# Opening of a banded attention + two-layer product kernel: the halves of v 0 later, the maxima of v shifted by a unit, w_in's transfer one pair earlier in the queue

## The reference, cut to what matters

```python
# attention: batch 2, heads 8, sequence 768, head width 64; n_global 8, n_local 96
scores = scale * q @ k.T + bias            # bias: -slope(head) * distance
scores = where(is_global | is_local, scores, -1e9)   # local: 0 <= row-col < 96; global: col < 8
a = softmax(scores);  x = a @ v            # fp32
x = reshape(x, (1536, 512))
h = x @ w_in (512 x 2048); g = h * tanh(softplus(h)); x = g @ w_out (2048 x 512)
p = domain_probs / sum(domain_probs)
out = sum over 4 experts e of p[:, e] * (relu(x @ w1[e]) @ w2[e])   # w1: 512 x 1024
```

## Time and profile before

| | us |
|---|---|
| median of 3 runs | 901.03 |
| lowest, highest | 900.47, 902.30 |
| the profiled execution's own time | 900.44 |
| its span in the trace | 898.5 |
| busy: PE, DVE, ACT, POOL | 872.5, 482.7, 319.0, 260.9 |

### The profile page before, as it was taken

The page is one execution under the profiler, slowest core; times in us unless marked ns, Lnnn a source line. Parts: engine busy times, 40 slices in busy tenths (PEclk is TensorE's granted clock), DMA queues, the critical chain, the costliest instruction groups (busy, mean ns, idle before and its releaser), DMA issues.

```text
span 898.5 us, 12643 instructions
## 1 busy us (share of the span) xinstructions
PE 872.5 (97%) x4918; PEld 444.0 (49%) x4918; DVE 482.7 (54%) x1008; ACT 319.0 (35%) x596; POOL 260.9 (29%) x222
## 2 busy tenths in 40 slices
PE   6988999999999999999999999999999999999998
PEld 5766876444444444444444444444444444444443
DVE  7756887999999989874442125222134321212121
ACT  4898886545554655542021010102010111101020
POOL 1659992222222222210039200077000292000000
PEclk8988999999999999999999999999999999999999
DMA  9961510000000000202100500001300000000001
GB/s 213 307 209 37 168 59 1 1 1 1 1 7 4 0 1 1 97 1 94 10 1 0 187 1 1 6 0 63 124 1 7 0 0 0 0 24 23 35 12 49
DMA packets 52004, 39.19 MB, mean 44 GB/s; under 512 B 40816, under 2 KB 41712, under 8 KB 51440
## 3 DMA queue, kind: packets, MB, share of 16 engines
q1 hardware_dynamic: 49888, 34.31, 12.9%
q10 hardware_dynamic: 2064, 4.19, 1.3%
HBM read 35.35 MB, written 3.15 MB: 43 GB/s over the span
## 4 chain that ended last, share of the span: by engine, by line
PE 89%; ACT 5%; DVE 3%; issue 1%; SPq 1%; DMA 0%; POOL 0%; DVEq 0%
PE bank L615 68%; PE bank L687 14%; PE bank L548 2%; PE bank L586 2%; ACT scaled L872 2%; PE bank L605 2%; ACT tmp L858 1%; ACT tmp L897 1%; PE bank L503 1%; DVE xT L1219 1%; SPq L420 1%; DMA xT<-in_v 0%; DVE tmp L1122 0%; ACT hid L848 0%; DVE tmp L1234 0%
## 5 line engine op out<-in xcount | busy, mean ns | idle before, releaser
L966 ACT ACTIVATE hid<-bank 128x512 f16<-128x512 f32 x96 | 57.3, 597 | 422.2 <-PE bank L615 422.2
L615 PE MATMUL bank<-xT,wA 128*128 128x512 f16 (+1 forms) x864 | 194.7, 379 | 0.0
L1344 DVE SCALAR_TENSOR_TENSOR hid<-bank,hid 128x512 f16<-128x512 f32 x96 | 66.4, 692 | 181.7 <-ACT hid L966 181.7
L615 PEld LDWEIGHTS bank<-xT,wA 128*128 128x128 f16 x864 | 84.4, 98 | 100.6
L687 PE MATMUL bank<-hid,wB 128*128 128x512 f16 x576 | 132.2, 379 | 0.9 <-DVE xT L1219 0.9
L615 PE MATMUL bank<-xT,wB 128*128 x576 | 125.3, 379 | 0.0
L615 PE MATMUL bank<-wB,hid 128*128 128x512 f16 x576 | 125.3, 379 | 0.0
L615 PE MATMUL bank<-wA,hid 128*128 128x512 f16 x576 | 125.3, 379 | 0.0
L824 POOL TENSOR_TENSOR tmp<-tmp 128x512 f32<-128x512 f32 x48 | 61.5, 1281 | 189.9 <-DVE tmp L1367 189.9
L781 POOL TENSOR_SCALAR stage<-stage,sc 128x1024 f32<-128x1024 f32 x32 | 36.0, 1125 | 260.4 <-DVEq L1337 250.4
L1424 DVE SCALAR_TENSOR_TENSOR acc<-bank,pg,acc 128x512 f32<-128x512 f32 x36 | 27.0, 750 | 131.7 <-PE bank L615 131.7
(11 more groups left out here) (113 smaller groups left out, 949.1 us busy)
## 6 DMA issues: line engine op xcount, KB each, us to landing
stage<-in_moe_w SPq DMA_DIRECT2D x8, 2048.0 KB, 9.8
stage<-in_moe_w_in SPq DMA_DIRECT2D x1, 4096.0 KB, 14.5
wB<-in_moe_w_out ACTq DMA_DIRECT2D x1, 4096.0 KB, 16.4
hid<-in_q SPq DMA_DIRECT2D x16, 192.0 KB, 3.4
hid<-in_k SPq DMA_DIRECT2D x16, 192.0 KB, 3.6
xT<-in_v SPq DMA_DIRECT2D x8, 384.0 KB, 5.1
out_y<-acc SPq DMA_DIRECT2D x12, 256.0 KB, 2.0
rows<-max SPq DMA_DIRECT2D x4, 128.0 KB, 4.3
```

Source lines behind the costliest of these rows:

```text
L615: last = pe.matmul(dst, lhs(c, a), rhs(c, b), start=(c == 0 and n == 0), stop=(c == chunks - 1 and n == 2))
L966: act.activation(hv[:, f, 0, :], psum(f % 4), ACT.Relu).then_inc(f_hi, 1)
L1344: dve.scalar_tensor_tensor(hv[:, f, 1, :], psum(f % 4), 0.0, hv[:, f, 0, :], ALU.max, ALU.subtract).then_inc(f_ready, 1)
```

## The change

Four things change; the arithmetic stays the same.

1. ACT's `values_high()` moves from ahead of pair 0 into unit 0 of pair 0, behind the high half of unit 0's P and the exponential of unit 2.
2. DVE's `values_low()` moves from ahead of pair 0 into unit 1, behind the low half of unit 1's P.
3. The maxima of v 1, 2, 4, 6 move from (ahead of pair 0, unit 1, unit 3, unit 5) to units 2, 3, 4 and 5.
4. SP issues w_in and the probabilities behind q and k of pair 2, ahead of those of pair 3.

```diff
         V_SUMS = list(range(3, PAIRS, 2))
+        V_MAX_AT = {2: 1, 3: 2, 4: 4, 5: 6}
+        VALUES_LOW_AT = 1
...
             for n in range(2, PAIRS):
                 sp.wait_ge(tr_psum, FILLS * (n - 1))
                 load_pair(n // 2, n % 2)
-                if n == 3:
+                if n == 2:
                     sp.dma_start(stage[:].rearrange("p (c f) -> p c f", c=DC), w_in_d).then_inc(w_loaded, 16)
...
                 if banded:
                     expo(0, 0, 0, banded)
                     expo(0, 0, 1, banded)
-                values_high()
+                else:
+                    values_high()
...
                     at = (2 * i + slot) * UNITS + u
+                    if banded and at == 0:
+                        values_high()
...
-            def value_step(u):
-
-                n = u + 1
-                if n < PAIRS and n not in V_SUMS:
+            def value_step(u, banded):
+
+                if banded and u == VALUES_LOW_AT:
+                    values_low()
+                if u in V_MAX_AT:
+                    n = V_MAX_AT[u]
                     dve.wait_ge(v_loaded[n], 16)
...
                 elif u + 1 == PAIRS:
-                    dve.wait_ge(v_pairs_max, PAIRS - 1 - len(V_SUMS))
+                    dve.wait_ge(v_pairs_max, len(V_MAX_AT))
...
-                value_step(0)
-                values_low()
-                pair(0, 0, is_banded, lambda u: u and value_step(u))
+                if not is_banded:
+                    values_low()
+                pair(0, 0, is_banded, lambda u: value_step(u, is_banded))
```

## The result

The changed kernel takes 906.94 us (median of 8 runs, 901.87 to 909.75), the kernel before 900.58 beside it (8 runs). The ratio is 1.0060, 95% interval 1.0046 to 1.0074: slower, by 6.4 us between the medians and 5.5 between the means. The forecast was 899.5, and the range (898.4 to 903.8) does not hold the time. The profiled execution took 906.68 with a span of 904.7, 6.2 longer than that of before.

What follows compares the result with a forecast made beforehand. PE, busy 97% of the span, was taken to bound the kernel, with engines in order so that opening savings reach the end. Opening -1.5 and w_in 0 on 901.03 gave 899.5 us, range 898.4 to 903.8.

Steps and rivals of the forecast that it cites:

- What bounds the kernel, and that opening time reaches the end: Whole kernel: PE busy 97%, engines in order; microseconds saved in the opening reach the end unless a transfer or POOL is late.
- The opening, -1.5: Pairs 0 and 1: reordering v 0's halves and the maxima saves 1.5 us, a little below the computed 1.73.
- timetable: Computed schedule of PE, ACT and DVE, unit 0 of pair 0 to pair 1's end: last unit 1.73 us early.
- w_in, 0: SP's queue: moving w_in and the probabilities ahead of pair 3's q and k was costed at 0 us.
- w_in through at 36.3, the probabilities at 37.5: SP's queue: times in us by which these transfers, issued from 24.3, would be through, before pair 3's packets.
- queued well ahead of w_out: SP's queue: pair 3's q and k are issued before w_out, so their possible 1.5 us loss was taken as 0.
- SP can keep the queue full: SP's queue: pair 2's transfers were taken to show this, as an argument against late q and k; no size.
- Some 1350 packets left at 39.2: Pair 3's packets when w_out's begin; sharing with w_out, they land near 47.7, past the allowed 46.2: 1.5 us lost.
- pair 3's q and k come late: Main rival, at pair 3's first fill: transfers stuck behind w_out land around 51; +3.3 us, 904.3; chance 0.25.
- most of its signs in the trace: Idle of several us before the fill near 45, ended by q or k; SP standing on L420 with w_out under way.
- The Trainium skill's rule: DMA engines alternate between queues by the packet, so small packets behind a second queue starve; it speaks against the change.

Runs made afterwards that it cites:

- e1: Parts 1 to 3 of the change on the kernel before, w_in and the probabilities back behind pair 3's q and k: 899.44 us for 901.19, ratio 0.9980.
- e8: The opening alone (parts 1 to 3 on the kernel before) repeated on another chip: 900.41 us for 900.89, ratio 0.9992.
- e11: The kernel before, unchanged, traced once more on another chip to see how it starts; no run time given.
- e12: The kernel before, unchanged, traced yet again to see how it starts; no run time given.
- e5: Parts 1 and 2 alone on the kernel before: v 0's halves moved, the maxima where they were; 902.25 us for 900.78, ratio 1.0008.
- e6: Part 3 alone on the kernel before: the maxima moved, v 0's halves still ahead of pair 0; 901.24 us for 900.78, ratio 1.0004.
- e2: Part 4 alone on the kernel before: w_in and the probabilities ahead of pair 3's q and k; 901.62 us for 901.19, ratio 1.0006.
- e3: The changed kernel with w_out issued four units later on ACT: 899.89 us where the kernel before has 901.19, ratio 0.9983.
- e4: The changed kernel with the probabilities back behind pair 3's q and k, only w_in ahead: 901.06 us where the kernel before has 901.19, ratio 1.0002.
- e10: The opening alone with 14 instead of 26 filler matmuls on PE ahead of the first fill: 900.99 us where the kernel before has 900.89, ratio 0.9995.

## Why the prediction was wrong

**What bounds the kernel, and that opening time reaches the end: right.** In e1's trace 1.5 us at pair 2's first fill (31.32 for 32.85) were still 1.5 at the first matmul group of w_out (165.69 for 167.20). A slow stretch of clock near 60 us can hide this: e8 is as early as e1 at pair 3's first fill (45.41), but has one and reaches w_out only at 167.37. The two traces of before that have one too (e11, e12) are there at 168.66, 1.3 later.

**The opening, -1.5: about right as a sum, wrong in its split.** Over the six traces that have the whole opening and all the fillers the scale of v comes at 28.25 to 28.96, over four that have the old one at 29.59 to 29.78, about 1.3 us apart; the runs give 1.25. The length of the wait at the first `pv` (1.92 us, timetable 1.9) and the order of the steps were as forecast. Wrong was that each part alone would give something: the timetable let e5 and e6 gain 0.6 and 0.4, they gained nothing.

**w_in, 0: wrong, and this is the step that failed.** The sum behind it had three terms, and I took its borderline result as nothing.
- w_in through at 36.3, the probabilities at 37.5: near enough. Most packets of the probabilities moved between 36 and 38.
- Pair 3's transfers "queued well ahead of w_out", since "SP can keep the queue full": this failed. I took it that q and k stand in the queue behind w_in and flow at 1040 packets per us once it is through. In fact SP was held 10.74 us on the second q and issued both k's at 38.28 and 38.87, level with w_out. The trace of before had a warning: SP's 9.07 us on two k's with w_out under way. It is not quite the same case, for there w_in was through and the 4 MB stood in ACT's queue. What the two have in common is that nothing or little of SP's small transfers moved while SP stood. I used that row for the rival and did not ask what it means for issues behind w_in.
- Some 1350 packets left at 39.2: it was both k's and most of the second q, about 2100. And they did not share from 39.2: SP's queue moved none from 41 to 43. So the last one landed at 54.7, not 47.7, and the loss was 9.4 us (54.76 for 45.36 in e1), not 1.5.

**The rival "pair 3's q and k come late" was right in its direction, its place (the fill near 45) and most of its signs in the trace.** Its way there was another: it let SP be stuck on the k's behind w_out, and landing at 51. SP was stuck on the second q behind w_in, before w_out was issued, and the k's themselves were issued in 0.55 and 0.84 us. I gave it 0.25 and priced it at +3.3; it was +6.4. The runs of the changed kernel spread from 901.87 to 909.75, those of the opening alone (e1 and e8) from 899.12 to 901.42 in 22. e2 with 0.8 us of start had 1.0 us of wait, e3 with 6.9 none. That the spread of single runs comes from how the race between 38.28 (k) and 38.31 (w_out) falls is argued from these, not traced.

**The Trainium skill's rule** ("DMA: Bandwidth & Descriptors", section "Queues, rings and completion order": the DMA engines take turns between queues by the packet) is what the trace after shows, 170 packets against 169. Two things beside it made the loss: SP stood while a large transfer was ahead in its queue, and for some 3 us SP's packets did not move at all behind a w_out just issued. The trace of before has that too: at 43:44, with SP's k's waiting, only w_out's queue moved.

```profile
q10 hardware_dynamic: 190, 0.39, 102.8%
```

**Left open.** What holds SP. e4 shows it is not the probabilities alone, since without them it stands 9.20 us one transfer later. A plain limit on the packets that wait in the queue does not fit both: e4 was held at the issue that makes 2304 packets behind w_in, the changed kernel passed 2304 (1536 of the probabilities, 768 of the first q) after 2.17 us and was held at 3072. In both, the one held is the third transfer issued behind w_in; no run here tests whether that is what counts. Nor was it tried whether the k's are held by the making of w_out's descriptors or by something in the DMA engines.

## What to carry to other kernels

A transfer that is moved ahead in a queue must be judged by what it delays and by what those will then meet, not by whether it is itself in time: here w_in was never late, before or after. 4 MB ahead of 0.8 MB made the kernel 6.4 us slower, and took the opening's gain besides, with another 4 MB issued at the moment when they were through. When those came 5.4 us later (e3), it cost next to nothing. If the engine that issues for a queue was seen standing on an issue in the trace of before, do not count the issues behind a large transfer as made at once: here SP stood 9 to 11 us, behind 4 MB in its own queue or beside 4 MB in another. Price steps that wait in line ahead of the same instruction together: here each part alone gave nothing, both about 1.3 us. For one of the two parts the reason is shown, for the other not.

## What the runs showed of the hardware that I had not expected

**The granted clock in the profile's rows can read 1.00 while the array is slow.** At 7:8 us, with PE busy with the same fillers and transposes, the trace of before has 11 matmuls and the trace after 7 (columns: PE busy, granted clock, DMA share, GB/s):

```profile
7.00:8.00 1.00, 1.00 (x11) 1.00 1.21 275
```

```profile
7.00:8.00 1.00, 1.00 (x7) 1.00 1.27 287
```

Twelve transposes take 1.47 us in most traces and 2.82 in e10, 1.9 times as long, both with a granted clock of 1.00 in the rows. So in the first microseconds the array runs at about half speed, and the moment when it speeds up differs from execution to execution: 26 fillers take 4.7 to 5.9 us, and the maximum of v 0 behind them begins anywhere from 10.87 to 12.24. With the old opening this shift is gone again by the scale of v (29.59 to 29.78 in four traces).

**Slow stretches later in attention move as well.** From the second fill issued in pair 2 to the first one in pair 3 the kernel before took 15.6 us in one execution and 17.2 in another (e12), there with the granted clock at 0.50 from 57 to 63. A difference of a microsecond between two single executions of this kernel says nothing.
